# Weight pieces handled in three steps, and product 3 accumulated in product 5's bank

## What is computed

```python
def _moe2_ref(x, U, V, w_ch1, w_ch2):      # x: 8 x 576 x 512, w_ch1: 512 x 2048, w_ch2: 2048 x 512
    xt = x.transpose(0, 2, 1)
    h = xt @ U @ V
    u = x + h.transpose(0, 2, 1)
    ch = np.maximum(u @ w_ch1, 0.0) @ w_ch2
    return (u + ch).astype(np.float32)
```

## Time and profile before

| quantity | value |
|---|---|
| median of 3 runs | 1481.69 us (1480.85 to 1483.5) |
| the profiled execution, its own time | 1482.97 us |
| its span, first to last instruction | 1480.9 us, so 2.07 us lie outside |
| PE busy | 1333.2 us, 90% of the span |
| mean granted TensorE clock | 0.967 of full speed |

### The profile page before, as it was taken

One profiled execution on the slowest core, in us unless ns is written; L12 is line 12 of the kernel. 1 busy time (PEld: TensorE's weight loads), 2 busy tenths in 40 slices (PEclk: granted clock), 3 DMA queues, 4 the chain that ended last, 5 costly groups with the idle time before them and its releaser, 6 DMA issues.

```text
span 1480.9 us, 21260 instructions
## 1 busy us (share of the span) xinstructions
PE 1333.2 (90%) x7592; PEld 1130.9 (76%) x7592; DVE 976.5 (66%) x1609; ACT 679.0 (46%) x1200; POOL 218.4 (15%) x294
## 2 busy tenths in 40 slices
PE   2379999999999996779978999999999999999996
PEld 1268787788878885668766878887788879899996
DVE  2767667666666655463667596857876587677766
ACT  1445464454545444344444454435444454354443
POOL 2700000000000036542354120002000010010000
PEclk9699999999999998889989999999999999999998
DMA  7744243323322036655689758875687668988986
GB/s 144 179 85 81 66 89 72 85 50 76 72 75 47 20 106 208 196 197 165 223 279 325 223 164 234 229 214 185 186 231 218 204 184 254 255 274 238 265 269 152
DMA packets 372456, 252.50 MB, mean 171 GB/s; under 512 B 249280, under 2 KB 286176, under 8 KB 372352
## 3 DMA queue, kind: packets, MB, share of 16 engines
q1 hardware_dynamic: 361056, 235.58, 56.6%
q0 software_dynamic: 4960, 13.79, 3.0%
q10 hardware_dynamic: 6336, 1.77, 0.6%
HBM read 201.25 MB, written 49.81 MB: 170 GB/s over the span
## 4 chain that ended last, share of the span: by engine, by line
PE 66%; DVE 13%; POOL 5%; SPq 5%; DMA 4%; ACT 4%; issue 3%; DVEq 0%; ACTq 0%; POOLq 0%
PE bank L1037 23%; PE bank L1119 17%; PE bank L779 10%; PE bank L793 8%; PE bank L758 3%; SPq L1289 3%; DVE mixed L731 2%; DVE hid_parts L1143 2%; DMA w_parts<-late_out 2%; DVE piece_out L1254 1%; DVE acc L1162 1%; PE bank L862 1%; DMA w_ring<-w_parts 1%; ACT piece_out L1249 1%; PE bank L932 1%
## 5 line engine op out<-in xcount | busy, mean ns | idle before, releaser
L1119 PE MATMUL bank<-hid_parts,w_ring 128*128 128x512 f32 (+1 forms) x1680 | 361.6, 371 | 17.1 <-DVE hid_parts L1143 7.5
L1037 PE MATMUL bank<-u_parts,w_ring 128*128 128x512 f32 (+1 forms) x1680 | 359.8, 372 | 10.4 <-DVE hid L1068 5.1
L1119 PEld LDWEIGHTS bank<-hid_parts,w_ring 128*128 128x128 f32 x1680 | 301.4, 188 | 75.8 <-issue 31.6
L1037 PEld LDWEIGHTS bank<-u_parts,w_ring 128*128 128x128 f32 x1680 | 309.0, 190 | 51.3 <-issue 12.2
L1137 ACT ACTIVATE hid_parts<-hid_raw 128x512 fp32r<-128x512 f32 (+1 forms) x280 | 164.0, 588 | 152.6 <-PE bank L1119 150.5
L1143 DVE TENSOR_TENSOR hid_parts<-hid_raw,hid_parts 128x512 fp32r<-128x512 f32 (+1 forms) x280 | 184.8, 665 | 47.5 <-ACT hid_parts L1137 43.9
L779 PE MATMUL bank<-xk_hi,wk_hi 128*128 128x384 f32 x384 | 132.8, 346 | 15.5 <-DVE xk_lo L750 8.7
L779 PE MATMUL bank<-xk_lo,wk_hi 128*128 128x384 f32 x384 | 130.3, 339 | 0.0
L779 PE MATMUL bank<-xk_hi,wk_lo 128*128 128x384 f32 x384 | 130.2, 339 | 0.0
L793 PE MATMUL bank<-wv_hi,k_hi 128*128 128x512 f32 x288 | 116.9, 406 | 1.1 <-DVE k_lo L829 1.1
L793 PE MATMUL bank<-wv_lo,k_hi 128*128 128x512 f32 x288 | 115.5, 401 | 0.0
(11 more groups left out here) (155 smaller groups left out, 1883.1 us busy)
## 6 DMA issues: line engine op xcount, KB each, us to landing
w_ring<-w_parts SPq DMA_DIRECT2D x560, 256.0 KB, 3.8
w_parts<-piece_out SPq DMA_DIRECT2D x20, 896.0 KB, 4.9
w_parts<-late_out SPq DMA_DIRECT2D x12, 896.0 KB, 6.3
x_scratch<-x SPq DMA_DIRECT2D x36, 256.0 KB, 2.0
kq_parts<-in_k SPq DMA_DIRECT2D x120, 72.0 KB, 2.5
kq_parts<-in_q SPq DMA_DIRECT2D x112, 72.0 KB, 2.2
v_rows<-in_v SPq DMA_DIRECT2D x56, 128.0 KB
out_dram<-acc SPq DMA_DIRECT2D x84, 64.0 KB, 3.1
```

The lines of the kernel that those rows point to most:

```text
L1037: last = nc.tensor.matmul(to, wring[:, e % RW, ct, a, :], uc[:, pos, b, ct, 0:w], start=(pos in FRESH and ct == 0 and a == 0 and b == 0), ...
L1119: last = nc.tensor.matmul(role(st, j, BANK_OF[pos])[:, 0:w], wring[:, e % RW, j, a, :], hid[:, no % RH, b, 0:w], start=(pos in FRESH and i ...
```

## The change

Four things are changed.

1. On POOL, the sums of piece n come before the load into the buffer that frees up (`pool_pieces`), where before the load stood first.
2. The items of a piece are taken apart: high part on ACT (`ws_hi`), low part on DVE one slot or spot later (`ws_lo`), store later still. In phase A piece n starts at slot 4 + 7n/5 instead of 4 + 3n/2, and its store comes three slots after instead of two. In phase B the spots in stage 2 are 3 entries apart instead of 4, and there are eight: the store of piece n-2, the low part of n-1 and the high part of n share a spot.
3. Product R22 (the scheme's product 3) is accumulated on bank Z, on top of T1 (product 5), instead of starting bank Y. So eb is a plain copy of bank X, and it moves from DVE to ACT; c12 adds bank Z. Stage 2 has 14 sums in a half instead of 16, two behind each product.
4. The roles alternate between two sets of banks instead of three, and the waits that guard the banks follow.

The buffers stay as they are: three and two output buffers, three and two raw buffers, 11 of w_ring, 3 of hid_parts.

```diff
     for n in range(PIECES - LATE):
-        at = 4 + 3 * n // 2
-        plan.setdefault(at, []).append(("ws_split", n))
-        plan.setdefault(at + 2, []).append(("ws_store", n))
+        at = 4 + 7 * n // 5
+        plan.setdefault(at, []).append(("ws_hi", n))
+        plan.setdefault(at + 1, []).append(("ws_lo", n))
+        plan.setdefault(at + 3, []).append(("ws_store", n))
...
-BANK_OF = "XZXYXYX"
-FRESH = (R11, T1, R21, R22)
-CHAIN = (T2, T3, T4)
+BANK_OF = "XZXYXZX"
+FRESH = (R11, T1, R21)
+CHAIN = (T2, T3, R22, T4)
...
-READY = {R11: SUMS[0:2], T1: SUMS[2:6], T2: SUMS[6:8], R21: SUMS[8:10], T3: SUMS[10:12], R22: SUMS[12:14],
-         T4: SUMS[14:16]}
+READY = {pos: SUMS[2 * pos:2 * pos + 2] for pos in range(NPROD)}
...
-LATE_SPOTS = [...] + [(1, 0, e) for e in range(3, 27, 4)]
+LATE_SPOTS = [...] + [(1, 0, e) for e in range(3, 19, 3)] + [(1, 0, 21), (1, 0, 24)]
...
-    items = [("ws_split", PIECES - LATE + at)]
-    if at > 0:
-        items.append(("ws_store", PIECES - LATE + at - 1))
+    items = []
+    for kind, after in (("ws_store", 2), ("ws_lo", 1), ("ws_hi", 0)):
+        if 0 <= at - after < LATE:
+            items.append((kind, PIECES - LATE + at - after))
...
-    trio = [{"X": (2, 3, 4), "Y": (4, 2, 3), "Z": (3, 4, 2)}, {"X": (5, 6, 7), "Y": (7, 5, 6), "Z": (6, 7, 5)}]
+    trio = [{"X": (2, 4), "Y": (4, 2), "Z": (3, 3)}, {"X": (7, 5), "Y": (5, 7), "Z": (6, 6)}]
...
         elif pos == R22:
-            pe.wait_ge(c11_ok, no + 1)
+            pe.wait_ge(p5_ok, no + 1)
...
+        elif kind == "eb":
+            act.wait_ge(prod_ps, entry(p, g, T2, i, 0) + 1)
+            ge(act, t_ok, 4 * no - 2)
+            nc.scalar.activation(hid_b[:, 0:w], role(st, side, "X")[:, 0:w], ACT.Copy).then_inc(b_ok, 1)
...
-        if kind == "eb":
-            dve.wait_ge(prod_ps, entry(p, g, T2, i, 0) + 1)
-            dve.wait_ge(p5_ok, no + 1)
-            nc.vector.tensor_tensor(hid_b[:, 0:w], of("X"), hid_z[:, 0:w], ALU.add).then_inc(b_ok, 1)
...
         for n in range(first, end):
+            pool_piece(pool, n)
             if n + slots - 1 < end:
                 if n > first:
                     pool.wait_ge(piece_lo, n)
                 load_piece(pool, n + slots - 1)
-            pool_piece(pool, n)
```

More of the change, by code:

```diff
@@ L218 @@
 NENTRY = NPROD * NU * 2 * NG * NB
-SUMS = [("11", "X", j) for j in range(2)] + [("12", "Z", j) for j in range(2)] + [("22", "Z", j) for j in range(2)] \
-    + [(out_, bank, j) for out_, bank in (("12", "X"), ("11", "Y"), ("22", "X"), ("12", "Y"), ("21", "X")) for j in range(2)]
+SUMS = [(out_, bank, j) for out_, bank in (("11", "X"), ("22", "Z"), ("12", "X"), ("11", "Y"), ("22", "X"), ("12", "Z"),
+                                           ("21", "X")) for j in range(2)]
 SUM_AT = {one: i for i, one in enumerate(SUMS)}
 NSUM = len(SUMS)
-READY = {R11: SUMS[0:2], T1: SUMS[2:6], T2: SUMS[6:8], R21: SUMS[8:10], T3: SUMS[10:12], R22: SUMS[12:14],
-         T4: SUMS[14:16]}
+READY = {pos: SUMS[2 * pos:2 * pos + 2] for pos in range(NPROD)}
 TILES = [("11", 0), ("11", 1), ("22", 0), ("22", 1), ("12", 0), ("12", 1), ("21", 0), ("21", 1)]
-LAST_SUM = {"11": "Y", "22": "X", "12": "Y", "21": "X"}
-LATE_SPOTS = [(0, 1, 1), (0, 1, 5), (0, 2, 2), (0, 2, 6), (0, 3, 1), (0, 3, 5)] + [(1, 0, e) for e in range(3, 27, 4)]
+LAST_SUM = {"11": "Y", "22": "X", "12": "Z", "21": "X"}
+LATE_SPOTS = [(0, 1, 1), (0, 1, 5), (0, 2, 2), (0, 2, 6), (0, 3, 1), (0, 3, 5)] + [(1, 0, e) for e in range(3, 19, 3)] + [(1, 0, 21), (1, 0, 24)]
 U_SPOTS = [(0, 1), (0, 4), (1, 1), (1, 4), (2, 5), (3, 1), (3, 3), (3, 5)]
@@ L285, in pair_plan @@
                 items += late_pieces((1, 0, e))
-            if p == 0 and g == 0 and e == NPROD * NU - 1:
-                items.append(("ws_store", PIECES - 1))
             if g == 0 and e in TURN_AT and turns:
@@ L455, in build @@
     u_bank = bank[0:2]
-    trio = [{"X": (2, 3, 4), "Y": (4, 2, 3), "Z": (3, 4, 2)}, {"X": (5, 6, 7), "Y": (7, 5, 6), "Z": (6, 7, 5)}]
+    trio = [{"X": (2, 4), "Y": (4, 2), "Z": (3, 3)}, {"X": (7, 5), "Y": (5, 7), "Z": (6, 6)}]
     def role(st, side, name):
-        return bank[trio[side][name][st % 3]]
+        return bank[trio[side][name][st % 2]]
     const_in, zeroed = sem("const_in"), sem("zeroed")
@@ L1012, in pe_m1 @@
             if st > 0:
-                last = {R11: ("22", "Z"), T1: ("12", "Y"), R21: ("21", "X")}[pos]
+                last = {R11: ("11", "Y"), T1: ("12", "Z"), R21: ("21", "X")}[pos]
                 pe.wait_ge(sum_ok, sum_no(p, g, 0) - NSUM + SUM_AT[last + (side,)] + 1)
-            elif (pos, i) == (R21, 1):
+            elif (pos, i) == (R11, 1):
                 pe.wait_ge(g_hi, B)
@@ L1022, in pe_m1 @@
         elif pos == T1:
-            pe.wait_ge(p5_ok, no - 1)
+            pe.wait_ge(c12_ok, no - 1)
         elif pos == R21:
-            pe.wait_ge(c12_ok, no - 1)
+            pe.wait_ge(c11_ok, no - 1)
         elif pos == T2:
@@ L1064, in dve_m1 @@
         of = lambda name: role(st, side, name)[:, 0:w]
-        if kind == "eb":
-            dve.wait_ge(prod_ps, entry(p, g, T2, i, 0) + 1)
-            dve.wait_ge(p5_ok, no + 1)
-            nc.vector.tensor_tensor(hid_b[:, 0:w], of("X"), hid_z[:, 0:w], ALU.add).then_inc(b_ok, 1)
-        elif kind == "c11":
+        if kind == "c11":
             dve.wait_ge(prod_ps, entry(p, g, R21, i, 0) + 1)
@@ L1081, in dve_m1 @@
             dve.wait_ge(b_ok, no + 1)
-            nc.vector.tensor_tensor(hid_b[:, 0:w], of("Y"), hid_b[:, 0:w], ALU.add).then_inc(c12_ok, 1)
+            nc.vector.tensor_tensor(hid_b[:, 0:w], of("Z"), hid_b[:, 0:w], ALU.add).then_inc(c12_ok, 1)
         elif kind == "t":
@@ L1114, in pe_m2 @@
             else:
-                before = {T2: R11, T3: T2, R22: R21, T4: T3}[pos]
-                pe.wait_ge(sum_ok, base + SUM_AT[READY[before][-1]] + 1)
+                read = {T2: R11, T3: T2, R22: T1, T4: T3}[pos]
+                pe.wait_ge(sum_ok, base + SUM_AT[READY[read][-1]] + 1)
         for j in range(2):
@@ L1662, in do_a @@
                 dve_us(dve, 0, item[2])
-            elif item[0] == "ws_split":
+            elif item[0] == "ws_lo":
                 dve_piece(dve, item[1])
         def do_b(item, p):
-            if item[0] in ("eb", "c11", "c22", "c12", "t"):
+            if item[0] in ("c11", "c22", "c12", "t"):
                 dve_m1(dve, item, p)
```

10 lines of the change are left out of this document (5 added, 5 removed).

## The result

The changed kernel takes **1504.76 us** (1503.87 to 1506.75), the kernel before 1481.73 on the same chip: the ratio is 1.0156, 95% interval 1.0138 to 1.0173. The profiled execution has a span of 1501.2 us, 20.3 more than before. The forecast was 1479, with a range up to 1496; the measured time lies 8.8 us beyond that end.

What follows compares the result with a forecast made beforehand. The prediction took PE, busy 90% of the span, as the bound. Its terms were -33 us (phase A), +36 (late pieces) and -6 (stage 2 of g = 1 and other stages), together -3: 1479 us, range 1462 to 1496.

Steps and rivals of the forecast that it cites:

- Place 1: Phase A while pieces are made, 540 to 662 us: of 43 us lost on PE 10 stay, so -33 us.
- the four sums: POOL's sums for one piece in phase A, taken at 2.4 us together, near the quiet end.
- 16 iterations: POOL's loop in phase A from piece 2 to piece 18: 64 us of loads and sums.
- the 0.93 of the earlier trace: Time in us of one POOL sum beside DVE work, taken to bound four sums at 3.7 us.
- 4 for ACT waiting on stores: Allowance in phase A: 4 us lost because the next user of a store's buffer stands closer behind it.
- The third rival: POOL's sums collide with DVE, 3.4 us for four: phase A gives 17 us instead of 33, total 1495; chance 0.10.
- Place 2: Late pieces in phase B, entries 17 to 55: high parts wait for stores issued later; +36 us, bounds +24 and +50.
- its round: Loop of one late spot in stage 2, from entry through store and high part back to PE: 10.9 us.
- the landing: Time for a late piece's store to land, within the loop of one spot: 6.1 us.
- the entry in the loop: The spot's own entry on PE, ahead of the store's issue: 1.37 us, plus 0.45 for the lower clock.
- Place 3: Stage 2 of g = 1 in each block with a successor, bound by DVE: 1.2 to 1.4 us saved in each of four.
- would cost up to 0.5 us a unit if an ACT wait stood ahead: Stage 1, eb moved to ACT: taken as covered since ACT is busy 46%, with this cost as the risk.

Runs made afterwards that it cites:

- plan_as_before: Changed kernel with phase A's plan as before (high and low part in one slot, pace 3/2, store two slots on): 1497.9 us, ratio 1.0066 to the kernel before.
- pace_alone: Changed kernel with early pieces' high and low part in one slot and store two slots on, as before; pace 7/5 kept: 1498.3 us, ratio 1.0085.
- late_store_ahead: Changed kernel with the store of each late piece one spot earlier, at the spot of its low part: 1486.4 us, ratio 1.0006 to the kernel before.
- before_sums_ahead: Kernel before with POOL's sums ahead of the next load, in both of POOL's loops, and nothing else: 1467.4 us, ratio 0.9879.
- eb_on_dve: Changed kernel with the copy eb back on DVE instead of ACT: 1498.9 us, ratio 1.0084 to the kernel before.
- one edit alone: Kernel before with POOL's sums ahead of the next load for the early pieces only, where there are three buffers: 1455.2 us, ratio 0.9795.

## Why the prediction was wrong

**Place 1, the step that failed.** Its sum read "the four sums ... I take 2.4, near the quiet end, since the present mean of 0.58 is already a mixture". The sums took 2.90 (560 to 640 us); by the prediction's own 16 iterations that is 8 us. The mean of before was taken while the order of work kept DVE idle during most sums; the edit itself ended that, since sums ahead of the load run beside whatever DVE does. Nor did the 0.93 of the earlier trace rows bound a sum: 1.30 was measured, and the trace of before has one of 1.19. The other part is a term that the prediction put at nothing: the low part moved a slot later. A load waits for it, and put back together with the store it gives 6 to 7 us (plan_as_before, pace_alone). The term that it did have for the plan, "4 for ACT waiting on stores", was large enough: 2.2 us of such waits were measured. 8 and 6 to 7 make up the 14.1 us by which place 1 fell short, as an estimate; it fits that kernels with the plan of before, whose sums are as long (2.96 to 3.01 us), gained 25 to 29 us in A, where the forecast of 33 less 9 for the sums would be 24. The third rival named the collision and gave 17 us for place 1 (18.9 measured), with a chance of 0.10; that its figure came so near is partly luck, since it took the sums at 3.4 us and had nothing for the low part either.

**Place 2 was right**, +36.0 for +36, in its mechanism (ACT's waits for w_parts<-late_out, groups of three entries, DMA share 0.64), its round (10.7 for 10.9) and its parts: +2.6 for +3 up to entry 31, +33.4 for +33 from there to entry 56. In the round two terms were off and cancelled: the landing was 5.1 to 5.5 us instead of 6.1, and the entry in the loop took 2.4 us in the mean instead of 1.37 and 0.45 for the clock. What the prediction did not see is a second loop behind the first: with the store early, 16 us stay (late_store_ahead), 8 of them from POOL's new order with two raw buffers (L of before_sums_ahead); the others are not taken apart. That edit was priced for place 1 only; for the late pieces it is a loss, which the waits for stores covered in the changed kernel.

**Place 3** was mis-sized and missed a wait. Stage 2 of g = 1 got shorter by 0.55 us a block (42.1 to 41.6) where 1.2 to 1.4 was forecast; why DVE's saved sums bring half is not tested. The step "would cost up to 0.5 us a unit if an ACT wait stood ahead" named the danger but not its size: one such wait for the output (4.12 us, the same copy, L950 there) was in the trace of before, where DVE had eb and PE lost nothing. With eb behind it, it cost 5.7 us at one place. eb_on_dve shows it.

**The sum.** -33 and +36 cancelled to -3, so the errors stand bare: 14.1 us in place 1, 7.0 in place 3 and the other stages (+1.0 for -6), and 2.2 ahead of phase A, where nothing was changed: 23.3, which is 20.3 less the forecast -3. The medians differ by 2.7 us more than the two profiled executions' spans. The range was drawn as if one term could fail at a time: the rival with 17 us for place 1 gave 1495, and 1496 was the end. Both failures have one form: an instruction moved to another place or engine meets what stands there, and that was priced by the trace of before, where it did not.

## What to carry to other kernels

Price an operation by what will run beside it after the change, not by its mean before; where a loop is opened, the engines that used to take turns now overlap. A wait that costs nothing today is the price of whatever is put behind it tomorrow, so before moving an instruction to an engine, list that engine's waits in every block, not only in the one that is being tuned. And an order that is good with three buffers (sum, then load) can be bad with two: run each part of a combined change by itself, since here one edit alone gave -2.0% and the bundle +1.6%.
